# Written-out batch loops, a different order of requests and mixing at the start of sweep two, and a last product in two banks

## The reference

```python
# attention in chunks of 32 queries, each against 8 memory rows and the keys from 16 before to 8 behind the chunk
scores = scale * np.matmul(q_c, k_full.transpose(0, 1, 3, 2))
a = np.exp(scores - max); a = a / (sum(a) + 1e-09)
out[:, :, c_start:c_end] = np.matmul(a, v_full)          # 8 heads of 64, x is [3072, 512]
# layer one
h = x @ w_in                                             # 512 -> 1024
sm = e / (np.sum(e) + 1e-09); solu = h * sm              # e = exp(h - max)
ln = (solu - mu) / np.sqrt(var + 1e-06) * g_ln
x = ln @ w_out                                           # 1024 -> 512
# layer two
h = x @ moe2_w_in                                        # 512 -> 2048
g = h * np.clip(h + 3.0, 0.0, 6.0) / 6.0
out = g @ moe2_w_out                                     # 2048 -> 512
```

## Time and profile before

| what | value |
|---|---|
| median of 3 runs | 946.51 us (946.47 to 947.03) |
| the profiled execution | 949.08 us, its span 947.3 us, mean granted clock 0.976 |
| PE busy | 902.4 us (95%), 6124 matmuls |
| DVE, ACT, POOL busy | 674.4, 471.2, 268.6 us |
| batches 0 to 3 and their tail | to about 444 us |
| sweep one | about 444 to 694.5 us |
| sweep two | about 694.5 us to the end |
| DMA | 146.84 MB, mean 155 GB/s |

### The profile page before, as it was taken

One profiled execution on the slowest core, in us unless ns is written; L12 is line 12 of the kernel. 1 busy time (PEld: TensorE's weight loads), 2 busy tenths in 40 slices (PEclk: granted clock), 3 DMA queues, 4 the chain that ended last, 5 costly groups with the idle time before them and its releaser, 6 DMA issues.

```text
span 947.3 us, 17198 instructions
## 1 busy us (share of the span) xinstructions
PE 902.4 (95%) x6124; PEld 807.5 (85%) x6124; DVE 674.4 (71%) x1097; ACT 471.2 (50%) x1092; POOL 268.6 (28%) x334
## 2 busy tenths in 40 slices
PE   6879999699997999999999999999999899999998
PEld 5768988589895888889978888888789899999997
DVE  3996878578774677857686555545777978878783
ACT  4675555355554565644675554555653333333320
POOL 3473355435331153462002332323540000000000
PEclk8999999799997999999999999999999999999999
DMA  9643365426743467359573333332987335344441
GB/s 183 143 117 82 79 179 168 153 59 158 221 137 104 100 180 199 122 154 329 190 256 118 127 133 133 129 137 106 341 323 265 117 109 157 97 149 123 140 140 45
DMA packets 146935, 146.84 MB, mean 155 GB/s; under 512 B 96936, under 2 KB 107176, under 8 KB 145832
## 3 DMA queue, kind: packets, MB, share of 16 engines
q1 hardware_dynamic: 133267, 100.29, 36.5%
q0 software_dynamic: 7920, 38.94, 11.7%
q10 hardware_dynamic: 5669, 6.56, 2.1%
HBM read 90.05 MB, written 55.71 MB: 154 GB/s over the span
## 4 chain that ended last, share of the span: by engine, by line
PE 85%; DVE 5%; DMA 5%; issue 3%; ACT 1%; POOL 0%; ACTq 0%; SPq 0%; DVEq 0%; POOLq 0%
PE banks L975 27%; PE banks L1240 23%; PE banks L1023 22%; PE banks L920 3%; PE banks L966 3%; PE banks L928 3%; PE banks L890 2%; PE banks L949 2%; DMA gs_raw<-g_scratch 2%; PE banks L990 1%; DMA ws<-w_split_scratch 1%; DMA xs_raw<-x_scratch 1%; DVE gs_raw L1878 1%; DVE prob L1586 1%; DVE gs L1547 1%
## 5 line engine op out<-in xcount | busy, mean ns | idle before, releaser
L1240 PE MATMUL banks<-vs,gs 128*128 128x256 f32 x2016 | 244.5, 284 | 3.6 <-DVE o_stage L1911 2.9
L1240 PEld LDWEIGHTS banks<-vs,gs 128*128 128x128 f32 x2016 | 243.7, 193 | 4.4 <-DVE o_stage L1911 3.1
L1023 PE MATMUL banks<-xs,ws 128*128 128x512 f32 x1008 | 231.3, 390 | 3.3 <-DMA ws<-w_split_scratch 2.3
L1023 PEld LDWEIGHTS banks<-xs,ws 128*128 128x128 f32 x1008 | 188.2, 188 | 45.0 <-DMA ws<-w_split_scratch 3.2
L1507 ACT CAST gs<-gs_raw 128x1792 fp32r<-128x1792 f32 x48 | 81.4, 1695 | 133.6 <-DVE gs_raw L1878 133.5
L975 PE MATMUL banks<-y_t,w_out 128*128 128x384 f32 x768 | 140.8, 338 | 0.0
L975 PEld LDWEIGHTS banks<-y_t,w_out 128*128 128x128 f32 x768 | 132.2, 188 | 0.7
L975 PE MATMUL banks<-w_in,x_t 128*128 128x512 f32 x504 | 122.5, 399 | 0.0
L975 PEld LDWEIGHTS banks<-w_in,x_t 128*128 128x128 f32 x504 | 94.8, 192 | 20.2
L1298 ACT ACTIVATE prob<-score,small 96x128 f32<-96x128 f32 x256 | 99.3, 392 | 18.7 <-DVE small L1564 17.8
L1878 DVE TENSOR_TENSOR gs_raw<-gs_raw 128x256 f32<-128x256 f32 x192 | 82.6, 431 | 31.6 <-DMA gs_raw<-g_scratch 26.6
(11 more groups left out here) (94 smaller groups left out, 1078.2 us busy)
## 6 DMA issues: line engine op xcount, KB each, us to landing
g_scratch<-part SPq DMA_DIRECT2D x96, 256.0 KB, 2.0
gs_raw<-g_scratch SPq DMA_DIRECT2D x45, 512.0 KB, 3.9
q_in<-in_q_dram SPq DMA_DIRECT2D x32, 192.0 KB, 4.1
x_scratch<-x_out ACTq DMA_DIRECT2D x32, 192.0 KB, 3.5
out_dram<-o_stage SPq DMA_DIRECT2D x12, 512.0 KB, 5.5
k_in<-in_k_dram SPq DMA_DIRECT2D x24, 240.0 KB
v_in<-in_v_dram SPq DMA_DIRECT2D x24, 240.0 KB
v_split_scratch<-v_split POOLq DMA_DIRECT2D x3, 1792.0 KB, 7.8
```

What stands on the lines that cost most here:

```text
L1023: mm = pe.matmul(ps, ws[:, W_OF[i], a, kc, :], xs[g][X_OF[i]][:, m, kc, :], start=(fresh and x == 0), stop=(x == len(passes) - 1), skip_gr ...
L1240: mm = pe.matmul(m_ps[i][:, s, :], gs[x][:, a, G_OF[i], s * P:(s + 1) * P], vs[p][:, m, V_OF[i], :], start=(p == 0 and s == 0 and y == 0), ...
```

## The change

Five engines' code is touched.

- On SP, PE, ACT and DVE (the diff shows SP's; the other three read alike) the hardware loop over batches 1 to 3 becomes a Python loop: the same body is written out three times, with constants in place of register values.
- POOL asks for V2 and V3 after it has made V0's low part, no longer together with V1.
- ACT rounds V2 behind the last unit of sweep one, no longer inside it; V3 directly behind V2, ahead of gs 2 and of the last relu; gs 4 ahead of V4.
- DVE makes V3's low part between the last sum and the last gate of sweep one, and mixes gs n+1 ahead of subtracting gs n also for n = 5 to 7 (before only from n = 8 on); gs 3 and gs 4 are mixed together, then both subtracted.
- In the last step the second half of product 3 (rows 128 to 255) goes to a PSUM bank of its own, so that DVE may add the first half while the second is computed. The seventh addition becomes two of 128x256, and the last 512 KB store becomes two of 256 KB, one on SP's queue and one on ACT's.

```diff
-            with sp.Fori(1, B) as b:
+            for b in range(1, B):
                 batch(b)
...
-            for h in (1, 0):
-                store_out(NGRP - 1, h)
-            for h in range(2):
-                sp.wait_ge(out_here[h], 16 * NGRP)
+            store_out(NGRP - 1, 1)
+            sp.wait_ge(m_summed, 7 * NGRP - 1)
+            sp.wait_ge(first_rows_summed, 1)
+            sp.dma_start(out[T - GT:T - GT + P, :], o_stage[:, 0, 0, :]).then_inc(out_here[0], 16)
+            sp.wait_ge(out_here[1], 16 * NGRP)
+            sp.wait_ge(out_here[0], 16 * (NGRP + 1))
...
-            for p in range(1, 4):
-                load_vs(p)
-            for p in range(VFIRST):
-                low_vs(p)
+            load_vs(1)
+            low_vs(0)
+            load_vs(2)
+            load_vs(3)
+            low_vs(1)
+            low_vs(2)
...
-                        mm = pe.matmul(m_ps[i][:, s, :], gs[x][:, a, G_OF[i], s * P:(s + 1) * P],
-                                       vs[p][:, m, V_OF[i], :], start=(p == 0 and s == 0 and y == 0),
+                        own_bank = grp == NGRP - 1 and i == M_ORDER[-1] and s == 1
+                        mm = pe.matmul(last_rows_ps if own_bank else m_ps[i][:, s, :],
+                                       gs[x][:, a, G_OF[i], s * P:(s + 1) * P], vs[p][:, m, V_OF[i], :],
+                                       start=(p == 0 and y == 0 and (s == 0 or own_bank)),
                                        stop=(p == PAIRS - 1 and y == 2), skip_group_check=True)
+                    if n == NGRP * PAIRS - 1 and i == M_ORDER[-1] and s == 0:
+                        mm.then_inc(last_product_begun, 1)
...
-            unit(PAIRS, 0, then={1: lambda: high_vs(1), 6: lambda: high_vs(2), 4: lambda: high_gs(2)})
+            unit(PAIRS, 0, then={1: lambda: high_vs(1)})
+            high_vs(2)
+            high_vs(3)
+            high_gs(2)
             relu_of(PAIRS, 0, 12)
...
             hold_first(NGRP - 1)
+            act.wait_ge(m_summed, 7 * NGRP)
+            act.dma_start(out[T - GT + P:T - GT + 2 * P, :], o_stage[:, 0, 1, :]).then_inc(out_here[0], 16)
...
             sum_of(PAIRS, 0, 12)
+            low_vs(3)
             gate(PAIRS, 0, 12)
...
-                add_product(grp, 3, c[12], s1)
+                if grp < NGRP - 1:
+                    add_product(grp, 3, c[12], s1)
+                else:
+                    dve.wait_ge(last_product_begun, 1)
+                    nc.vector.scalar_tensor_tensor(out=c[12][:, 0, :], in0=m_ps[3][:, 0, :], scalar=SIXTH,
+                                                   in1=s1[:, 0, :], op0=ALU.mult, op1=ALU.add
+                                                   ).then_inc(first_rows_summed, 1)
+                    dve.wait_ge(m_done[3], NGRP)
+                    nc.vector.scalar_tensor_tensor(out=c[12][:, 1, :], in0=last_rows_ps, scalar=SIXTH,
+                                                   in1=s1[:, 1, :], op0=ALU.mult, op1=ALU.add
+                                                   ).then_inc(m_summed, 1)
```

More of the change, by code:

```diff
@@ L172, in attention_solu_hardswish @@
         M_BANK = {1: 1, 2: 6, 6: 5, 7: 2, 4: 7, 5: 4, 3: 0}
+        last_rows_ps = banks[:, 3, 0:GH]
         m_ps = {i: banks[:, M_BANK[i], :].rearrange("p (s n) -> p s n", s=2) for i in M_BANK}
@@ L205, in attention_solu_hardswish @@
         out_here = [sem(f"out_here{h}") for h in range(2)]
+        last_product_begun = sem("last_product_begun")
+        first_rows_summed = sem("first_rows_summed")
         cleared = sem("cleared")
@@ L1172, in _ @@
             first_batch()
-            with pe.Fori(1, B) as b:
+            for b in range(1, B):
                 batch(b)
@@ L1475, in _ @@
             first_batch()
-            with act.Fori(1, B) as b:
+            for b in range(1, B):
                 batch(b)
@@ L1529, in _ @@
             unit(last, 2, then={1: lambda: high_gs(0), 6: lambda: high_vs(0), 7: lambda: high_gs(1)})
-            unit(PAIRS, 0, then={1: lambda: high_vs(1), 6: lambda: high_vs(2), 4: lambda: high_gs(2)})
+            unit(PAIRS, 0, then={1: lambda: high_vs(1)})
+            high_vs(2)
+            high_vs(3)
+            high_gs(2)
             relu_of(PAIRS, 0, 12)
             high_gs(3)
-            for n in range(3, PAIRS):
-                if n < VLATE:
-                    high_vs(n)
-                high_gs(n + 1)
+            high_gs(4)
+            high_vs(4)
+            for n in range(5, PAIRS + 1):
+                high_gs(n)
             for n in range(PAIRS + 1, NGRP * PAIRS):
@@ L1834, in _ @@
             first_batch()
-            with dve.Fori(1, B) as b:
+            for b in range(1, B):
                 batch(b)
@@ L1904, in _ @@
             sum_of(PAIRS, 0, 12)
+            low_vs(3)
             gate(PAIRS, 0, 12)
+            low_gs(2)
             mix_gs(3)
-            low_gs(2)
+            mix_gs(4)
+            low_gs(3)
+            low_gs(4)
+            low_vs(4)
+            mix_gs(5)
             def add_product(grp, i, to, of):
@@ L1935, in finish @@
                 dve.wait_ge(m_summed, done + 6)
-                add_product(grp, 3, c[12], s1)
-            for n in range(3, PAIRS):
-                low_gs(n)
-                mix_gs(n + 1)
-                if n < VLATE:
-                    low_vs(n)
-            for n in range(PAIRS, NGRP * PAIRS):
+                if grp < NGRP - 1:
[9 more added lines that the diff above has]
+                                                   ).then_inc(m_summed, 1)
+            for n in range(5, NGRP * PAIRS):
                 if n + 1 < NGRP * PAIRS:
@@ L1946, in _ @@
                 low_gs(n)
-                if n % PAIRS == 1:
+                if n % PAIRS == 1 and n > PAIRS:
                     finish(n // PAIRS - 1)
```

## The result

The changed kernel takes 922.98 us (median of 4 runs, 922.70 to 923.57). The kernel before, run beside it, takes 946.77 (4 runs, 946.47 to 951.45). The ratio is 0.9738, 95% interval 0.9708 to 0.9769: 2.6% faster.

A forecast was written before the change was run, and what follows sets the result against it. PE, 95% busy, was taken as the bound, stopped or slowed at the seams, sweep turn and end. 22.6 + 2.1 + 0.5 = 25.2 us off 946.51 (the profile's 2.57 us above median carried over) gave 921.3 us, range 918.8 to 927.

The forecast's parts named there:

- Part one: At the two seams between batch passes, writing out the loops removes PE's stops and half-clock time: 22.6 us less.
- Below nothing it can't go far: Bound on the seams' gain: the step can't take much less than its 4.91 us of matmuls; 0.5 us kept.
- Part two: At the turn from sweep one to sweep two, moved requests and reordered mixing and rounding gain 2.1 us.
- Sweep one ends 1.7 us earlier: At sweep one's end the ws waits go, leaving a new 0.9 us wait for ACT; end at 692.9.
- The cover of 2 us for V2: Before sweep two's step 2, POOL finishes V2's low part at 701, 2 us before PE needs it at 703.2.
- the wait of 3.3 us ahead of step 6: In sweep two PE waits 3.3 us for gs, because mixing gs 7 now stands ahead of subtracting gs 6.
- the loss behind the 2.93 us gap: In sweep two, after PE's wait for `finish`'s first addition, the lower clock costs 1.65 us over 71 matmuls.
- Part three: At the kernel's end, two half additions and smaller last stores move the end from 946.9 to 946.4: 0.5 us less.
- One (the DMA crowd): Seam stops come from crowded DMAs, not the jump, and stay; only 2.6 us go, 943.9 us; chance 0.04.
- Two (a stop a seam stays): Code comes late in written-out batches too, one stop a seam; 14 of 22.6 us stay, 935; chance 0.09.
- Three (every packet missed): Without loops PE meets each 16 KB code packet as new, at least 3.4 us each; all missed 979 us; chance 0.02.
- Four: At sweep two's start, mixing order costs more than ws blocks give: 1 to 2 us worse, 924.5; inside the forecast's 0.83.

The follow-up runs named there:

- e3: Kernel before with only PE's batch loop written out, SP, ACT and DVE still jumping back; 941.56 us, ratio 0.9929.
- e4: Changed kernel with PE's short hardware loop in sweep one written out too; 923.05 us, ratio 0.9737.
- e7: Changed kernel with the end as before: last product in one bank, one full seventh addition, one last 512 KB store; 922.64 us, ratio 0.9735.
- e11: Changed kernel with V7 requested behind gs 7 instead of ahead of it; 923.31 us, ratio 0.9733.
- e9: Kernel before with only the four batch loops written out, the same kernel as e1 run again on another group's chip; 923.01 us, ratio 0.9738.
- e1: Kernel before with only the batch loops of SP, PE, ACT and DVE written out; 925.45 us, ratio 0.9762.
- e5: Changed kernel with POOL asking for V1, V2 and V3 together again, as before; 922.83 us, ratio 0.9725.
- e2: Changed kernel with the four batch loops put back as hardware loops; 947.31 us, ratio 0.9995.
- e10: The changed kernel itself, run again beside the third group; 922.56 us, ratio 0.9738.
- e6: Changed kernel with mixing and low parts of gs 5 to 7 in the order of before; 925.26 us, ratio 0.9752.
- e12: e5 with V7 requested behind gs 7 instead of ahead of it; 921.64 us, ratio 0.9717.

## Why the prediction was right, point by point

**What bounds the kernel.** Right. The "issue" rows at the seams were the jump back, on PE and on ACT (e3), the packets of q8 stand in PE's stops, and the short loop pays nothing (e4). That all engines stop for themselves is shown for PE and ACT only.

**Part one: 22.6 forecast, 24.4 measured on the chain.** The first hidden products of the passes stood at 76.17, 189.71, 302.43 and 405.75 and now stand at 76.43, 178.37, 280.04 and 381.64: 329.58 - 305.21 = 24.4 us. The mechanism is right; the term was mis-sized by its norm, the undisturbed step. I took the exit of the loop (4.91 us from turning q to the hidden product) as the undisturbed step, and it takes 4.35 at the written-out seam. That 0.56 us counts three times, at both seams and at the exit itself. The "Below nothing it can't go far" bound of 0.5 us counted matmuls of a step that was itself slow. The hole named there, the missing loads of q and k, was none: with them the step is faster. Of the 24.4 us, 24.0 are left at C.

**Part two: 2.1 forecast, 1.5 between the two profiles, nothing on average.** The first step that failed is "Sweep one ends 1.7 us earlier". It ended later: sweep two begins 19.8 us after C instead of 18.1 (672.21 and 694.48), and 18.9 where the clock stayed up (e4, e7, e11). The ws waits went and ACT's wait came (0.9 forecast, 1.06 measured), but DVE's gate grew from 1.1 to 4.3 us. I had moved POOL's work in time without asking which DVE operations it would now stand beside. The cover of 2 us for V2 failed with it: POOL's seven pieces took 9.77 us, not 6.8, beside DVE's work, and the wait for V2 before step 2, which I had named as a sign of being wrong, is there with 1.12 us in e4, e7 and e11. In the changed kernel's first profile only the slower clock hides it. The second is the wait of 3.3 us ahead of step 6. It was 0.43 us, since PE came there later and gs 7 came no earlier than its bytes allow. The third is the clock: I priced the loss behind the 2.93 us gap at 1.65 us. From step 8's second product to F it takes 199.15 us before (939.13 - 739.98) and 198.29 after (913.63 - 715.34), so the difference is 0.86, with a new wait of 0.35 us for DVE in the second. And no limit between 1.8 and 2.9 us, as I had put it, decides on the clock: it fell after PE had stood for 1.78 us in e3, 2.13 here and 2.23 in e9, and stayed up after 2.36 in e1, 2.35 in e5 and 2.13 in e7. The fourth is the one that matters most: the 2.93 us wait was a property of that one execution. Three more executions with the same code there (e1, e3, e9) took 260.45 to 261.78 us from C to F, the changed kernel and its like (e2, e4, e7, e10) 261.09 to 261.27. The mean of either set is 261.2, and that of the order of before is 261.6 if its first profile is counted too. So part two gives 0.4 us at most, which no run resolves. What it may do is make the turn steadier: 0.2 us between its five profiles, 2.3 between the four with the order of before. That is few profiles to say it from.

Within part two the runs separate the pieces in part: mixing ahead is worth 2.4 to 2.7 us once the requests are moved (e6), and the moved requests give nothing that shows (e5; e11 against e12). Why POOL shuts DVE out in its row for V1, while the 21 pieces in a row let gates of 1.1 us in between, stays open.

**Part three: 0.5 forecast, 0.1 measured.** The additions came as forecast, halves of 0.42 and 0.41 us. The term that was mis-sized is the last landing, which I had put at the 2.2 us of SP's queue. SP's store did take 2.2, but it carries the first half. The second half's store goes out last, on ACT's queue at 918.64, 0.44 us after its addition began, and lands in 2.6 us, where the last store before took 2.8. So the smaller store saves 0.2 us of landing and not 0.6. The 0.1 us lies within the bounds named.

**The sum and its base.** 25.2 against 25.5 for the profiled executions. The rest of the miss is the step "I carry that over": the profile of before stood 2.57 us above its median, that of after 0.6 above, and so the median gained only 23.8. What set the profile of before off its median isn't shown. The stops alone vary by less between two profiles (seam one takes 16.12 us before and 16.63 in e2, seam two 14.27 and 14.76). A difference taken from one profile belongs to that profile.

**The rivals.** One (the DMA crowd) would leave the stops; they are gone in e1, where POOL and SP issue the same DMAs, and e2 brings them back. Two (a stop a seam stays) falls with the 0.11 us row. Three (every packet missed) falls with PE's chain and the queue's 44 packets. Four gave 924.5, and the start of sweep two did lose what it was to give; but the mixing order, which the rival blamed, is the piece that gains, and the moved requests bring the long gate.

## What to carry to other kernels

Where several engines show "issue" gaps of microseconds after the jump back of a long loop, write the loop out on all of them at once: PE's alone gave 6.3 of 22.4 us here, since ACT still stopped. Whether SP and DVE need it wasn't tried. Leave short loops alone. Before moving work of POOL in time, list the DVE operations with two SBUF inputs that it will stand beside, and take effects of 1 to 2 us from several executions, measured between two events that the edit leaves alone.

## What was not expected of the hardware

- One DVE operation of 1.1 us took 4.30 or 4.31 us in seven profiles, beside a row of POOL instructions of 0.70 us each (4.89 us for 7), and ended 0.54 or 0.55 us behind the row each time.
- ACT's stop after the jump back is longer than a single one of PE's: 8.68 us at the first seam in e3, where PE's stops at that seam in e2 are 2.80 to 3.12 us each.
- The length of a pause alone doesn't say whether TensorE's clock falls to 1.2 GHz. Busy times by stretch behind the ws wait, in which PE had stood for 2.36 us in e1 (first row) and 2.23 us in e9 (second row):

```profile
666.00:668.00 2.00, 1.88 (x8) 1.58 (x9) 0.94 (x2) 1.67 (x2) 2.00 (x4) 1.00 1.05 406
```

```profile
662.00:664.00 2.00, 1.85 (x5) 1.47 (x6) 0.87 (x1) 1.78 (x2) 2.00 (x3) 0.59 1.05 405
```

The longer pause kept the clock, the shorter one lost it. And behind the wait of 2.08 to 2.13 us for DVE's sum, the same in seven profiles, the clock fell in four (the changed kernel, e2, e6, e10) and stayed up in three (e4, e7, e11). What decides wasn't tried.
